# Attention, mixture of experts and mixer on one core: where TensorE turns the rows and logits of a finished batch

## The reference, cut to what matters

```
batch, n_heads, seq, head_dim = (4, 8, 576, 64)

# attention, per batch and head: pooled branch + local branch
q_d = q.reshape(B, H, 144, 4, D).mean(axis=3)         # the same for k, v
out_up = np.repeat(sm_attn(q_d, k_d, v_d), 4, axis=2)
mask = np.abs(pos[:, None] - pos[None, :]) < 4        # a band of 7 keys
out_local = softmax(where(mask, scale * q @ k.T, -1e9)) @ v
x = (out_up + out_local), laid out as [4, 576, 512]

# routing
logits = einsum('bsd,de->bse', x, w_gate)             # 8 experts
local_gate = sigmoid(einsum('bsd,de->bse', x, w_local))
# per token: the expert of argmax(logits) if local_gate < 0.5 or s == 0,
# else the expert of the token before; out = p[e] * (relu(x @ w1[e]) @ w2[e])
```

## Time and profile before

| | us |
|---|---|
| median of 3 runs | 888.42 |
| the runs | 884.23, 888.42, 890.13 |
| the profiled execution | 888.59 |
| its span in the trace | 886.9 |
| TensorE busy | 849.8 (96%) |
| VectorE, ScalarE, GpSimd busy | 390.6, 335.1, 217.1 |
| hb 2 (57.49 to 81.15) | 23.66 |
| hb 3, hb 5 | 17.16 each |
| hb 4, hb 6 | 25.10, 25.11 |

### The profile page before, as it was taken

One profiled execution on the slowest core, in us unless ns is written; L12 is line 12 of the kernel. 1 busy time (PEld: TensorE's weight loads), 2 busy tenths in 40 slices (PEclk: granted clock), 3 DMA queues, 4 the chain that ended last, 5 costly groups with the idle time before them and its releaser, 6 DMA issues.

```text
span 886.9 us, 14421 instructions
## 1 busy us (share of the span) xinstructions
PE 849.8 (96%) x5089; PEld 698.7 (79%) x5090; DVE 390.6 (44%) x781; ACT 335.1 (38%) x858; POOL 217.1 (24%) x325
## 2 busy tenths in 40 slices
PE   5999998988998999999999999999999999999998
PEld 3777666654787888888788758999999889999997
DVE  2577877756643533456645265112222252121211
ACT  4577777752452524355635251111112121111110
POOL 5688888734221121212212100000000000000000
PEclk9999999997999999999999999999999999999999
DMA  9669788511637432555545240001020200000100
GB/s 163 112 111 212 173 212 177 172 50 30 224 115 233 156 122 83 189 170 198 185 159 168 81 166 1 1 1 72 1 72 0 72 1 1 1 36 1 36 0 36
DMA packets 94130, 88.49 MB, mean 100 GB/s; under 512 B 63213, under 2 KB 68991, under 8 KB 94079
## 3 DMA queue, kind: packets, MB, share of 16 engines
q1 hardware_dynamic: 90203, 75.21, 30.7%
q0 software_dynamic: 3840, 12.59, 4.3%
q10 hardware_dynamic: 36, 0.01, 0.0%
HBM read 72.31 MB, written 15.48 MB: 99 GB/s over the span
## 4 chain that ended last, share of the span: by engine, by line
PE 78%; POOL 6%; DMA 5%; DVE 4%; issue 3%; ACT 2%; SPq 1%; ACTq 0%; DVEq 0%; POOLq 0%
PE scores L1626 11%; PE scores L1627 11%; PE scores L1628 11%; PE bank L1628 6%; PE bank L1626 6%; PE bank L1627 6%; PE bank L1678 4%; PE bank L1679 4%; PE bank L1685 4%; POOL asb L732 2%; DMA stage<-in_moe_w 2%; DMA v<-in_v 2%; PE scores L1499 2%; PE scores L1669 1%; PE bank L1426 1%
## 5 line engine op out<-in xcount | busy, mean ns | idle before, releaser
L1348 DVE SCALAR_TENSOR_TENSOR h2l<-scores,h2h 128x384 fp32r<-128x384 f32 x72 | 40.2, 558 | 192.2 <-ACT h2h L1013 192.2
L1013 ACT ACTIVATE h2h<-scores 128x384 fp32r<-128x384 f32 x72 | 35.4, 492 | 229.8 <-PE scores L1628 229.8
L1626 PE MATMUL scores<-uTh,W 128*128 128x384 f32 x288 | 98.1, 341 | 0.0
L1627 PE MATMUL scores<-uTl,W 128*128 128x384 f32 x288 | 97.5, 338 | 0.0
L1628 PE MATMUL scores<-uTh,W 128*128 128x384 f32 x288 | 97.3, 338 | 0.0
L1628 PE MATMUL bank<-W,h2l 128*128 128x512 f32 x216 | 84.5, 391 | 0.0
L1626 PE MATMUL bank<-W,h2h 128*128 128x512 f32 x216 | 84.3, 390 | 0.0
L1627 PE MATMUL bank<-W,h2h 128*128 128x512 f32 x216 | 84.0, 389 | 0.0
L1286 DVE TENSOR_TENSOR W<-stage,W 128x1024 fp32r<-128x1024 f32 x56 | 66.7, 1221 | 27.1 <-ACT W L959 24.6
L959 ACT ACTIVATE W<-stage 128x1024 fp32r<-128x1024 f32 x56 | 57.8, 1054 | 51.7 <-DVE ysb L1304 24.3
L1678 PE MATMUL bank<-W,hTh 128*128 128x512 f32 x184 | 76.3, 415 | 0.0
(11 more groups left out here) (236 smaller groups left out, 1651.4 us busy)
## 6 DMA issues: line engine op xcount, KB each, us to landing
stage<-in_moe_w SPq DMA_DIRECT2D x56, 512.0 KB, 4.5
vl<-in_v SPq DMA_DIRECT2D x40, 128.0 KB, 3.6
qraw<-in_q SPq DMA_DIRECT2D x32, 144.0 KB, 5.6
kraw<-in_k SPq DMA_DIRECT2D x32, 144.0 KB, 5.1
v<-in_v SPq DMA_DIRECT2D x8, 576.0 KB
ub<-y_dr SPq DMA_DIRECT2D x18, 256.0 KB, 4.4
out<-ob SPq DMA_DIRECT2D x18, 256.0 KB, 2.1
x_dr<-xrow SPq DMA_DIRECT2D x16, 256.0 KB, 3.6
```

Of the source, the lines that this page charges most:

```text
L1013: act.activation(dst, bank[bk][:, 0:width], ACT.Relu).then_inc(relu_hi, 1)
L1348: dve.scalar_tensor_tensor(dst, bank[bk][:, 0:width], 0.0, hi.bitcast(F32), ALU.max, ALU.subtract).then_inc(bank_free, 1)
L1626: pe.matmul(ps, ah, bh, start=first, stop=False)
L1627: pe.matmul(ps, ah, bl, start=False, stop=False)
```

## The change

In steps 0 to 71 the pieces of a step are issued at two places: the turns where they were, right behind the scores, and the rows, logits and turned logits at the end of the step, behind `turn_probs` and `weigh`. From step 72 on there are no turns and the rest stays where it was. The lists, the banks, the semaphores and the other engines' programs are the same.

```diff
--- before.py
+++ after.py
@@ -1557,8 +1557,11 @@
                     pe.matmul(bk[:, :].rearrange("p (r c) -> p r c", r=4), ones_b[:, :],
                               bc(ident_b[:, :].unsqueeze(1), [P, 4, P]), start=True, stop=True)
 
-            def side_pieces(g):
+            def side_pieces(g, of_units):
+
                 for kind, a, i in side_work(g):
+                    if (kind == "turn") != of_units:
+                        continue
                     if kind == "turn":
                         turn(a, i)
                     elif kind == "rows":
@@ -1574,7 +1577,7 @@
                 if g < NU:
                     scores(g)
                 if g < NU:
-                    side_pieces(g)
+                    side_pieces(g, True)
                 if 0 <= g - 3 < NU:
                     turn_probs(g - 3)
                 if 0 <= g - 4 < NU:
@@ -1583,8 +1586,7 @@
                     pe.wait_ge(route_const, 1)
                     keep_busy(3, bank[5])
                     turn_marks()
-                if g >= NU:
-                    side_pieces(g)
+                side_pieces(g, False)
 
             for j in range(2):
                 pe.wait_ge(side_free[j], (len(SIDE) + 1 - j) // 2)
```

## The result

The changed kernel takes 894.41 us (median of 20 runs, 887.87 to 898.46) against 885.81 us of the kernel before in the same comparison (20 runs, 881.83 to 890.13): ratio 1.0091, 95% interval 1.0075 to 1.0106. The two medians differ by 8.6 us. The forecast was 889.0 with a range up to 892.0. It stood on a median of three runs, 888.42, which lies 2.6 us above that of the twenty, so the step from one kernel to the other was missed by 8.0 us (8.6 for 0.6). Ratios and intervals come from the fast runs of both kernels; of all kernels in this document that leaves out one run, 897.63 us in experiment 4.

A forecast was written before the change was run, and what follows sets the result against it. In even half batches no engine is full; TensorE, in program order, meets short waits. Half-batch terms summed to +0.62 us on the median 888.42, giving 889.0 us, range 885.0 to 892.0.

The forecast's parts named there:

- rival 4: Longer u2 wait drops TensorE's clock through one even half batch: slower beyond 1%, 904.5 us; chance 0.04.
- 16 us: Claimed growth of one even half batch's 22.05 us of TensorE work if all ran at the low clock.
- waits of 0.95 stand in hb 4 with granted 1.00: Argument against a clock fall: half batch 4 already had 0.95 us waits at full granted clock.
- My table of waits: TensorE waits, half batches 2 to 7: 2.9 us for GpSimd, 2.8 + 0.5 for ScalarE, 1.7 for VectorE.
- The sum of the order: Reordering costs 0.01 us in half batch 2, 0.20 each in 4 and 6, 0.21 in 7: total +0.62.
- Loss (a): At u2 of half batch 2 the piece covered a GpSimd wait; moving it makes the next scores 0.38 us later.
- the losses at u2 and u3: Half batch 4: scores after u2 come 0.44 us late; after u3 still 0.44 late, not 0.88.
- the lost gain: In half batches 4 and 6, the gain at u6 gives nothing because turn(u7) waits on ScalarE's chain.
- the gain at u5: Half batch 4: piece no longer waits for ScalarE to empty its bank, saving 0.13 us.
- rival 2: Earlier weighing removes the 3.3 us of attention waits for ScalarE and losses are absorbed: 884.6 us; chance 0.14.
- rival 3: Small unabsorbed losses plus ScalarE's copy uncovered once each in half batches 4 and 6: +3.2, 891.6 us; chance 0.10.
- No GpSimd instruction moves: Claim, among edits costed at nothing, that GpSimd's instructions stay in place across the attention.

The follow-up runs named there:

- experiment 4: Kernel before with only the three u2 rows pieces moved behind the weighing: 889.59 us, ratio 1.0010.
- experiment 1: Changed kernel with a second, unsent copy of each u2 rows piece at its old place, filling the wait: 888.72 us, ratio 1.0017.
- experiment 2: Changed kernel with the three u2 rows pieces kept at their old place: 886.45 us, ratio 0.9989.
- experiment 7: Changed kernel with the u2 rows pieces kept and one weight split moved from half batch 4 to 7: 887.04 us, ratio 1.0026.
- experiment 3: Changed kernel with one weight split moved from u5 of half batch 4 to u6 of half batch 7: 890.17 us, ratio 1.0045.
- experiment 5: Changed kernel with the three u3 rows pieces kept at their old place: 891.13 us, ratio 1.0069.
- experiment 12: Changed kernel with four unread matmuls ahead of turn_probs at u1 of half batches 1, 2, 4 and 6: 888.81 us, ratio 1.0028.
- experiment 9: Kernel before with ten unread early matmuls and four-matmul fillers misplaced at steps other than u1: 885.81 us, ratio 0.9997.
- experiment 11: Changed kernel with four-matmul fillers meant for u1 but misplaced at other steps: 887.62 us, ratio 1.0013.
- experiment 8: Kernel before with ten unread matmuls added in steps 1 and 3 as a warm start: 885.37 us, ratio 0.9988.

## Why the prediction was wrong

**The failed step is the chance given to rival 4**, the fall of the clock: 0.04. It had named what happened: the wait at u2 grew from 0.18 to 0.62, as measured, the clock fell in an even half batch, and its score matmuls took 1.21 us. Its price of 16 us was too high. Its picture, the lengthened wait setting off the fall on the spot, was too simple: in the profiled run the clock fell 0.4 us before that wait began. What the runs show is a rate: with the wait at u2 filled or its piece kept everywhere, 0 of 36 runs are low (experiments 1, 2, 7); with it left open and the wait at u1 unfilled, 14 of 20, 5 of 12, 3 of 12 and 3 of 9 (changed kernel, experiments 3 to 5); with it left open and the wait at u1 filled, 0 of 12 (experiment 12). I set the rival aside because "waits of 0.95 stand in hb 4 with granted 1.00". That row shows one wait in one execution, and a place like it did see falls later (experiments 4 and 9). What the runs point to is how idle stretches stand together: 0.91, 0.20 and 0.18 at u1 and u2 left the clock up in nearly all runs before; with 0.90 to 1.14, 0.20 and 0.62 a quarter to seven tenths of the runs are low. My table of waits gave totals and hid that the one I lengthened begins 2.4 us behind the end of the longest wait for the same engine (144.92 to 147.28). The Trainium skill's rule ("TensorE: Matmul & The Clock Gate", section "Why this matters for your kernels"), cited there as speaking against the change, told the direction; I let one counter-example in the trace outweigh it. The runs bear out its advice to leave no idle gaps (experiments 1 and 12). The gaps it warns of there are longer than any that did harm here (at most 1.14 us), so by its letter it would not have forecast this fall.

**The price.** All TensorE work of half batch 6 at the low level was to cost 16 us. It cost 8.8: busy time grew by 9.84 (31.90 - 22.06), as the fall began 6.1 us into the half batch and ended before the next, and idle time shrank by 1.07 (3.05 to 1.98), since a slow TensorE waits for nobody. Of the 9.13 us at the end of the attention, 3.3 came back in the first expert.

**The sum of the order came out, its terms in part by luck.** Forecast 0.01 for half batch 2, 0.20 for 4, 0.21 for 7, and nothing for the odd ones. Measured: half batch 6 starts 0.21 later (140.57 to 140.78), made up of 0.04 at the start of half batch 4, 0.10 in it and 0.07 behind it. Half batch 7 and the close take 17.81 for 17.66, +0.15. Half batch 2 itself is 0.08 longer (23.74 for 23.66). Loss (a) held: at u2 of half batch 2 turn_probs starts 0.68 behind the turn where 0.30 is free, so 0.38 late. In half batch 4 the losses at u2 and u3 held too (turn(u5) comes 0.44 later), but I had put the lost gain in the wrong step: turn(u6), not turn(u7), waits on ScalarE's chain, so the gain at u5 vanished in that wait (0.20 became 0.38), and those at u6 and u7 counted, 0.35 together for my 0.24. The waits for ScalarE in half batch 4 did not shrink (0.95 became 1.02 at u5), so rival 2 did not come about, and ScalarE's exponentials at u5 follow its xrow copy at the same distance as before (0.53), so rival 3 did not either. Changed kernels without a low run stand at 0.9989 to 1.0028 (experiments 1, 2, 7, 11, 12, with their fillers and kept pieces), -1.0 to +2.5 us, around the 0.6 of the sum: the order's own cost is not resolved.

**What the sum had no term for**: the weight split that met GpSimd, with 0.41 us less between their starts. "No GpSimd instruction moves" was true of the order, not of the time.

**Open:** what share of falls the collision adds; why the same waits let the clock fall in one half batch and not in the next (experiment 4); why in the changed kernel's trace it fell before the wait at u2, at a point up to which experiments 1 and 2 read alike and stayed up; how the rate differs from chip to chip; and where the falls of the untraced runs lie, the 4 of 119 of the kernel before among them.

## What to carry to other kernels

Work that stands ahead of a wait may be keeping the clock up as well as filling time: before moving it, list the idle stretches of TensorE in order of time and look for those that come to stand close together, instead of adding them up by cause. Price the fall by its likelihood over many runs, for one trace with full clock is one draw. Where a short wait can't be removed, unread matmuls in it can be worth their price: experiment 12 has no low run and stands 0.3% above the kernel before, where the changed kernel stands 0.9% above it. A warm start alone gained nothing that could be told; with the waits at u1 filled it gained 0.5%.

## What the runs showed of the hardware that I had not expected

The clock fell with TensorE far from idle: in the 5 us before it fell in the changed kernel's trace (141.92 to 146.92) TensorE was busy for 3.67 us, and its longest gap was 1.14 us.

The granted clock of the profile is no witness early on. Window and timeline of the kernel before:

```profile
25.00:30.00 5.00, 5.00 (x38) 3.85 (x35) 2.27 (x7) 2.08 (x9) 2.97 (x5) 1.00 1.20 183
```

```profile
28.09 1.21 PE L1499 MATMUL scores<-kT,qT 64*120 64x128 f32 x8
```

It reads 1.00 there, while eight score matmuls take 1.21 us; in experiment 8 they take 0.70 from 20 us on. The duration of a matmul of known shape is the safer reading.

A kernel's time can have two humps: the changed one has six runs at 887.9 to 891.0 (mean clock 0.985 to 0.992) and fourteen at 892.5 to 898.5 (0.977 to 0.981). A median of three runs of such a kernel could be either.
